# Attention inside a two-layer expert kernel: five TensorE visits a step in place of eight, and the outer product by head

## The reference

```python
for t in range(S):                                   # B, H, S, D = 4, 8, 768, 48
    cur = einsum('bhd,bhe->bhde', u * k[t], v[t])
    y[t] = einsum('bhd,bhde->bhe', r[t], state + cur)
    state = w[t][..., None] * state + einsum('bhd,bhe->bhde', k[t], v[t])
x = y.transpose(0, 2, 1, 3).reshape(B * S, H * D)    # 3072 x 384
h = x @ w_in;  x = (h * clip(h + 3, 0, 6) / 6) @ w_out     # d_ff = 2048
h = x @ w_in2; x = (h / (1 + exp(-h))) @ w_out2
```

## Time and profile before

| | |
|---|---|
| median of the runs | 945.53 us |
| the profiled execution | 945.16 us, its span 943.4 us |
| PE busy | 916.1 us (97%) |
| PEld, DVE, ACT, POOL busy | 84%, 49%, 33%, 16% |
| mean granted clock of TensorE | 0.978 |
| of the chain that ended last | PE 93%, DVE 2% |

### The profile page before, as it was taken

The page is one execution under the profiler, slowest core; times in us unless marked ns, Lnnn a source line. Parts: engine busy times, 40 slices in busy tenths (PEclk is TensorE's granted clock), DMA queues, the critical chain, the costliest instruction groups (busy, mean ns, idle before and its releaser), DMA issues.

```text
span 943.4 us, 14944 instructions
## 1 busy us (share of the span) xinstructions
PE 916.1 (97%) x5684; PEld 788.7 (84%) x5684; DVE 457.7 (49%) x692; ACT 313.9 (33%) x517; POOL 148.8 (16%) x134
## 2 busy tenths in 40 slices
PE   5679999999999999999999999999999999999998
PEld 4568888888888888888888789999999999999997
DVE  6866646564664656466445643333333333343332
ACT  2343223233223323332244542333332332332332
POOL 6454213321421332142000000000000000000000
PEclk7679999999999999999999999999999999999999
DMA  7561130304113030311203100000000000000000
GB/s 239 189 175 56 56 98 12 109 0 109 54 54 88 20 109 0 109 54 54 100 1 101 67 1 0 15 19 0 33 0 0 33 0 0 33 0 0 34 1 34
DMA packets 13367, 48.54 MB, mean 51 GB/s; under 512 B 1568, under 2 KB 2208, under 8 KB 13344
## 3 DMA queue, kind: packets, MB, share of 16 engines
q1 hardware_dynamic: 13344, 48.23, 16.3%
HBM read 43.50 MB, written 4.72 MB: 51 GB/s over the span
## 4 chain that ended last, share of the span: by engine, by line
PE 93%; DVE 2%; DMA 1%; POOL 1%; issue 1%; ACT 0%; SPq 0%; POOLq 0%; ACTq 0%
PE bank L652 15%; PE bank L653 14%; PE bank L654 14%; PE bank L676 7%; PE bank L678 7%; PE bank L677 7%; PE bank L664 7%; PE bank L666 7%; PE bank L665 7%; PE bank L706 2%; PE bank L732 2%; PE bank L716 2%; PE bank L736 1%; DMA x<-u_row 1%; PE bank L698 1%
## 5 line engine op out<-in xcount | busy, mean ns | idle before, releaser
L652 PE MATMUL bank<-x_hi,w_hi 128*128 (+1 forms) x576 | 230.0, 399 | 1.4 <-DVE x_lo L563 1.4
L654 PE MATMUL bank<-x_hi,w_lo 128*128 (+1 forms) x576 | 227.1, 394 | 0.0
L653 PE MATMUL bank<-x_lo,w_hi 128*128 (+1 forms) x576 | 227.0, 394 | 0.0
L375 ACT CAST g_hi<-g 128x512 fp32r<-128x512 f32 x192 | 119.1, 620 | 286.3 <-PE bank L678 144.3
L491 DVE TENSOR_TENSOR g<-g,bank 128x512 f32<-128x512 f32 x96 | 66.0, 687 | 244.4 <-ACT g L369 244.4
L498 DVE TENSOR_TENSOR g_lo<-g,g_hi 128x512 fp32r<-128x512 f32 x192 | 138.3, 720 | 0.9 <-ACT g_hi L375 0.9
L493 DVE SCALAR_TENSOR_TENSOR g<-g,bank 128x512 f32<-128x512 f32 x96 | 66.0, 688 | 141.3 <-ACT g L367 141.3
L652 PEld LDWEIGHTS bank<-x_hi,w_hi 128*128 128x128 f32 x576 | 108.8, 189 | 27.2 <-issue 4.0
L678 PE MATMUL bank<-w_hi,g_lo 128*128 128x384 f32 x384 | 129.5, 337 | 0.0
L676 PE MATMUL bank<-w_hi,g_hi 128*128 128x384 f32 x384 | 129.5, 337 | 0.0
L677 PE MATMUL bank<-w_lo,g_hi 128*128 128x384 f32 x384 | 128.9, 336 | 0.0
(11 more groups left out here) (89 smaller groups left out, 817.6 us busy)
## 6 DMA issues: line engine op xcount, KB each, us to landing
unit_in<-rkv_tm SPq DMA_DIRECT2D x23, 576.0 KB, 6.5
unit_in<-rk_fm SPq DMA_DIRECT2D x23, 448.0 KB, 4.1
x<-w SPq DMA_DIRECT2D x8, 768.0 KB, 4.9
unit_in<-w SPq DMA_DIRECT2D x8, 768.0 KB, 4.4
unit_in<-w_fm SPq DMA_DIRECT2D x23, 226.2 KB, 2.9
out<-tmp SPq DMA_DIRECT2D x5, 768.0 KB, 3.3
out<-tmp SPq DMA_DIRECT2D x4, 192.0 KB, 2.0
x<-rkv_tm SPq DMA_DIRECT2D x1, 576.0 KB, 12.7
```

The lines of the kernel that those rows point to most:

```text
L375: nc.scalar.copy(g_hi[:, p, :], g[:, p, :]).then_inc(ghi_done, 1)
L652: nc.tensor.matmul(h_ps[j % 2][:, :], wh, xh, start=k == 0, stop=False)
L653: nc.tensor.matmul(h_ps[j % 2][:, :], wh, xl, start=False, stop=False)
L654: last = nc.tensor.matmul(h_ps[j % 2][:, :], wl, xh, start=False, stop=k == KT - 1)
```

## The change

The pieces get names, and two that held two things are parted: transposes (TURN) and scores (SCORES), outer product (OUTER) and values (VALUES). `RUN_SLOTS` gives way to `VISITS = [3, 6, 9, 12, 14]`. Visit 0 does transposes and scores of unit 0. Visits 1 to 3 (the middle visits) do the transposes of unit b, outer product and values of unit b-1, and then the scores of unit b. Visit 4 does outer product and values of unit 3. The two scans of a unit stand in the slot ahead of its visit, its row sums in the visit. The transposes share `att[1]` with scores, the outer product shares `att[0]` with scores, the output has `att[2]`. Scores therefore wait for the copied keys (`kt_kept`) and for the addition of unit b-1's outer product to its state (`added`), and that addition now waits for the state's last read (`state_read`). On GpSimd the two products come behind decayed keys and queries; a one-column multiplication (`spin`) takes the waits ahead of the diagonal. The outer product is 8 matmuls of 48 columns, even heads at partitions 0 to 47 and odd heads at 64 to 111, in place of 4 of 96 over 112 rows, half of whose results were not used. The prologue keeps its order, apart from the outer product's form.

```diff
@@ -121,7 +122,7 @@
...
-        run_banks = [[att[0], att[1], att[2], att[2], att[0]]]
+        run_banks = [[att[0], att[1], att[0], att[1], att[2]]]
         pro_banks = [att + bank[3:5], bank[0:3] + bank[3:5]]
...
@@ -204,9 +207,13 @@
...
+        SCAN, FORWARD, OWN, TURN, SCORES, MASK, OUTER, VALUES, STATE, XHI, XLO = range(11)
+
         def pro_pieces(slot):
-            order = ([(0, 0), (0, 5), (1, 0), (1, 5)] if slot == 0 else
-                     [(slot - 1, 4), (slot - 1, 1), (slot - 2, 2), (slot - 2, 3), (slot + 1, 0), (slot + 1, 5)])
+            order = ([(0, SCAN), (0, FORWARD), (1, SCAN), (1, FORWARD)] if slot == 0 else
+                     [(slot - 1, OWN), (slot - 1, TURN), (slot - 1, SCORES), (slot - 1, MASK),
+                      (slot - 2, OUTER), (slot - 2, VALUES), (slot - 2, STATE), (slot - 2, XHI), (slot - 2, XLO),
+                      (slot + 1, SCAN), (slot + 1, FORWARD)])
             return [(b, k) for b, k in order if 0 <= b < B]
...
@@ -216,10 +223,17 @@
...
-        RUN_SLOTS = {0: 2, 4: 2, 5: 3, 1: 4, 2: 5, 3: 5}
+        VISITS = [3, 6, 9, 12, 14]
         def run_pieces(slot):
-            return [(b, k) for k, first in RUN_SLOTS.items() for b in range(B) if slot == 3 * b + first]
+            pieces = []
+            if slot in VISITS:
+                b = VISITS.index(slot)
+                pieces = [(b, OWN), (b, TURN), (b - 1, OUTER), (b - 1, VALUES), (b - 1, STATE), (b, SCORES), (b - 1, XHI), (b - 1, XLO), (b, MASK)]
+            elif slot + 1 in VISITS:
+                b = VISITS.index(slot + 1)
+                pieces = [(b, SCAN), (b, FORWARD)]
+            return [(b, k) for b, k in pieces if 0 <= b < B]
...
@@ -327,11 +341,10 @@
...
-            def queries_and_diagonal(b, a, c):
+            def old_diagonal_read(b, a, c):
                 pool.wait_ge(own_done, a + 1)
                 pool.wait_ge(y_full, a)
-                decayed_queries(b, a, c)
-                own_diagonal(b, a, c)
+                nc.gpsimd.tensor_tensor(spin[:, :], half[:, :], half[:, :], ALU.mult).then_inc(spun, 1)
...
@@ -352,9 +365,11 @@
...
                 for b in range(B):
+                    decayed_keys(b, B * (c + 1) + b, c)
+                    decayed_queries(b, B * (c + 1) + b, c)
                     own_products(b, B * (c + 1) + b, c)
-                    decayed_keys(b, B * (c + 1) + b, c)
-                    queries_and_diagonal(b, B * (c + 1) + b, c)
+                    old_diagonal_read(b, B * (c + 1) + b, c)
+                    own_diagonal(b, B * (c + 1) + b, c)
...
@@ -512,22 +527,22 @@
...
                     p_last = segs(back)[:, :, 0:1]
-                    if k == 0:
+                    if k == SCAN:
                         dve.wait_ge(w_loaded[m], 16 * taken(b, c))
...
                         if c is not None:
-                            dve.wait_ge(scaled, 2 * (a - B))
+                            dve.wait_ge(masked, 2 * a)
                         nc.vector.tensor_tensor_scan(back[:, ::-1], w[:, 1:WSEG][:, ::-1], back_add[:, ::-1], 0.0,
...
                         nc.vector.reciprocal(segs(fwd_add[:, :])[:, :, 0:1], p_last).then_inc(start_done, 1)
-                    if k == 5:
+                    if k == FORWARD:
                         dve.wait_ge(start_done, a + 1)
                         nc.vector.tensor_tensor_scan(fwd[:, :], w[:, 0:PAIRS * SEG], fwd_add[:, :], 0.0, ALU.mult, ALU.add).then_inc(fwd_done, 1)
-                    if k == 1:
+                    if k == MASK:
                         dve.wait_ge(diag_done, a + 1)
...
@@ -538,27 +553,27 @@
...
                                                       banks[q][:, :].rearrange("p (h t) -> p h t", h=4)).then_inc(masked, 1)
-                    if k == 4:
+                    if k == OWN:
                         dve.wait_ge(rku_done, a + 1)
...
                                              tm[:, 0, :].rearrange("p (i q d) -> p i q d", i=PAIRS, q=2), AX.X).then_inc(own_done, 1)
-                    if k == 2:
+                    if k == STATE:
                         if c is None:
...
                         else:
-                            dve.wait_ge(y_full, a + 1)
+                            dve.wait_ge(state_read, a - B + 1)
                             dve.wait_ge(scaled, 2 * (a - B) + 2)
-                        outer = banks[2][:, 0:PAIRS * 2 * D].rearrange("p (i e) -> p i e", i=PAIRS)
+                        outer = banks[2][:, 0:PAIRS * D].rearrange("p (i e) -> p i e", i=PAIRS)
                         for odd in range(2):
...
                             if c is None:
-                                nc.vector.tensor_copy(st, outer[rows, :, cols]).then_inc(added, 1)
+                                nc.vector.tensor_copy(st, outer[rows, :, :]).then_inc(added, 1)
                             else:
-                                nc.vector.tensor_tensor(st, st, outer[rows, :, cols], ALU.add).then_inc(added, 1)
-                    if k == 3:
+                                nc.vector.tensor_tensor(st, st, outer[rows, :, :], ALU.add).then_inc(added, 1)
+                    if k == XLO:
                         dve.wait_ge(xhi_done, a + 1)
...
@@ -688,18 +703,20 @@
...
                     rk, w, tm = units[m]
-                    if k == 1:
+                    if k == TURN:
                         pe.wait_ge(kt_done, a + 1)
                         if sets == 1:
-                            pe.wait_ge(added, 2 * a)
+                            pe.wait_ge(masked, 2 * a)
                         elif a > 0:
...
                         last.then_inc(kt_turned, 1)
+                    if k == SCORES:
                         pe.wait_ge(rt_done, a + 1)
                         if sets == 1:
-                            pe.wait_ge(xlo_done, a)
+                            pe.wait_ge(kt_kept, a + 1)
+                            pe.wait_ge(added, 2 * a)
                         for h in range(H):
...
@@ -707,15 +724,20 @@
...
                                 last.then_inc(scores_full, 1)
-                    if k == 2:
+                    if k == OUTER:
                         pe.wait_ge(kt_kept, a + 1)
-                        if some(2 * (a + 1 - sets)):
+                        if sets == 1:
+                            pe.wait_ge(masked, 2 * a + 2)
+                        elif a + 1 > sets:
                             pe.wait_ge(added, 2 * (a + 1 - sets))
                         pe.wait_ge(tm_loaded[m], 16 * taken(b, c))
-                        for i in range(PAIRS):
-                            last = nc.tensor.matmul(banks[2][0:KROWS, i * 2 * D:(i + 1) * 2 * D], kt_tok[:, i * KROWS:(i + 1) * KROWS],
-                                                    tm[:, 2, i * 2 * D:(i + 1) * 2 * D], start=True, stop=True)
+                        for h in range(H):
+                            q, i = h % 2, h // 2
+                            last = nc.tensor.matmul(banks[2][ODD * q:ODD * q + D, i * D:(i + 1) * D],
+                                                    kt_tok[:, i * KROWS + ODD * q:i * KROWS + ODD * q + D],
+                                                    tm[:, 2, h * D:(h + 1) * D], start=True, stop=True)
                         last.then_inc(outer_full, 1)
+                    if k == VALUES:
                         x_bank = banks[4]
...
@@ -729,7 +751,8 @@
...
                                 i, e = n // 3, n % 3 * Q
-                                nc.tensor.matmul(region(n), state[b][0:KROWS, i, e:e + Q], rk[:, 0, i, :], start=n < 4, stop=False)
+                                last = nc.tensor.matmul(region(n), state[b][0:KROWS, i, e:e + Q], rk[:, 0, i, :], start=n < 4, stop=False)
+                            last.then_inc(state_read, 1)
                         for n in range(REGIONS):
...
```

More of the change, by code:

```diff
@@ L74, in build @@
         half = sb("half", [P, 1])
+        spin = sb("spin", [P, 1])
         def x2_step(c, k):
@@ L150, in build @@
         scaled = sem("scaled")
+        state_read = sem("state_read")
         added = sem("added")
@@ L164, in build @@
         diag_done = sem("diag_done")
+        spun = sem("spun")
         v_mid_done = sem("v_mid_done")
@@ L406, in attention @@
                         nc.scalar.copy(v_mid_put[b % 2], middle.rearrange("p i (q e) -> p i q e", q=2)).then_inc(v_mid_done, 1)
-                    if k == 3:
+                    if k == XHI:
                         act.wait_ge(y_full, a + 1)
```

## The result

The changed kernel takes 983.15 us (median of 4 runs, 981.89 to 985.09) against 946.18 us: a ratio of 1.0394, 95% interval 1.0365 to 1.0423, slower. The forecast was 985 in a range of 955 to 1000. The profiled execution has a span of 980.3 us, and of the chain that ended last TensorE now holds 78% where it held 93%.

The account below looks back on a forecast made before the run. TensorE bounds the kernel, so attention costs the time TensorE spends on it. A step adds 3 x 1.58 + 1.09 - 0.22 = 5.61 us, five 28.0, on 945.16 gives 973.2; 12 for the clock gives 985, range 955 to 1000.

Parts of the forecast that it names:

- Three exits a step: Delays of the dense matmuls behind an attention visit on TensorE, taken at 0.16 us each; joining visits removes three a step.
- The term of 0.028 a record: Outer product: 0.028 us per narrow record, from the values' rows, so 16 take 0.45; a gain beyond 0.45 was excluded.
- T: Zero point of the forecast's times: the end of `sums1` in the visit's slot.
- 4.42: TensorE's cost in us of one attention unit in the kernel before: 1.57 + 2.53 + 0.32.
- Each station: Chain before middle-visit scores: backward scan, keys, forward scan, queries, `g_lo`, two products, row sums, additions; scores at T + 4.75.
- the scan's meeting with the keys: VectorE's forward scan, held up by GpSimd's decayed keys on the shared port pair, ends 1.09 us behind them.
- The meetings of `g_lo` with queries and product: `g_lo` on VectorE ends 0.54 us after GpSimd's queries; the first product takes 1.43 and ends 0.86 after `g_lo`.
- two rows: Clock evidence: 2.8 us of standing before 45.40 brought clock 0.50; a 0.7 us pause at 539 left it 1.00.
- The clock kept at 973: Rival 1: the same waits with TensorE's clock kept, 973 us (968 to 978); chance 0.26.
- harmless meetings at 953: Rival 2: the two port-pair meetings don't lengthen the chain, 1.5 us a step, 953 (949 to 960); chance 0.13.
- the clock lost nearly everywhere: Rival 4: clock lost in nearly every visit or slow to return, 24 to 33 us over 973, 997 to 1006; chance 0.09.
- The faster side: Rival 3: additions come in time for scores, 937 us, or 941 with visit 0's copy waited for; chance 0.07.

Follow-up runs that it names:

- the outer product alone: The kernel before with only the outer product's new form, 8 matmuls of 48 columns in two column halves: 940.26 us, 0.9937.
- two experiments from different sides: Changed kernel with products ahead of keys and queries again: 944.45 us; changed kernel with backward scans of units 1 to 3 a slot earlier: 944.03 us.
- a third: Changed kernel with GpSimd's decayed keys in the loop cut to one column per pair: 958.23 us, 1.0122.
- The filled pause: Changed kernel with seven more matmuls of 512 columns in each middle visit, ahead of the wait for the addition: 970.21 us, 1.0252.
- unit 0's own bank alone: Changed kernel with only the transposes of unit 0 moved to `att[2]`, so its scores skip the wait for the keys' copy: 982.05 us, 1.0377.
- joined, no pause: Changed kernel with visits in slots 4, 7, 10, 13, 14, backward scans two slots ahead, forward scans one, unit 0's transposes in `att[2]`: 938.66 us, 0.9923.

## Why the prediction was right

**What it saves.** Three exits a step and the outer product. The last visit saved 0.29 and not 0.22 (the same 0.29 a unit as with the outer product alone): L736 to L754 is 0.49 with the change of tiles, where I had 0.55, and the 0.09 for the entry came as forecast. The term of 0.028 a record was taken from 128-column streams; with 48 columns it is about (0.49 - 0.10) / 16 = 0.024. By that the bound I had excluded (faster than 0.028) was crossed.

**The middle visits.** Forecast 1.58 us more for each, without the clock: scores at T + 4.75. Measured: the visits end 5.69 after T on average with 0.14 to 0.15 behind, 5.84 in all, 1.42 more than 4.42. Each station was in its place. The additions ended at T + 4.45 in the visit shown, 0.25 ahead of the forecast: 0.13 by the second product (0.87 for 1.00) and 0.12 along the way to it. (The forecast's own terms add up to T + 4.75 for their end, not 4.70; row sums and additions overlap by about as much in the trace.) Of this, 0.10 is given back because scores start 0.15 behind the additions and not 0.05. That the products' place decides is shown by two experiments from different sides, that the scan's meeting with the keys lengthens the chain, by a third: without it the scores came 0.82 us earlier on average. The meetings of `g_lo` with queries and product were only read from the trace, where their ends fit to 0.02 us.

**Visit 0.** Forecast 1.09, measured 2.49 + 0.17 + 0.15 (a late `g_lo` two slots on, in four of the five turns) against 1.73: 1.08. For the masks it took 2.3 us, where its rows give 2.2 and the trace has 2.15.

**The clock.** Forecast: half of the 15 visits at 1.6 us. Measured: 8, at 5.8 - 4.2 = 1.6. The filled pause gives the same 12.9 us by itself. This was the term with the widest bounds (0 to 33), and that it fell in the middle was a guess between two rows; the loss doesn't go by the pause's length (a visit with scores at T + 4.40 lost the clock, one with T + 4.72 kept it). The count is the profiled run's. The mean granted clock of the four runs is 0.964 to 0.969 and lowest in the two slowest, so it was probably not 8 in each; with unit 0's own bank alone it was 7 of 15. The size was a choice too: the clock was at 0.50 in both rows from 45.40 to 51.80, and the forecast priced one of them; behind the middle visit shown it was at 0.50 for one such stretch, 88.40 to 91.60.

**The sum.** 15 x 1.42 + 5 x 1.08 - 5 x 0.29 + 8 x 1.6 = 38.1 us, and the five turns of the loop show just 38.1. The start of the loop was 1.1 us earlier than in the trace of before, which makes 980.4 for a span of 980.3. Forecast were 28.0 + 12 = 40.

**Joined visits.** The prediction gave the three exits 0.48 us a step; the expectations of later runs held that the change of tile shapes takes this back. By the steps 81.91 (separate, outer product by head) and 81.64 (joined, no pause) joining is worth 0.26 us a step, 1.3 us in 938. What takes the rest back is not the tiles: a middle visit takes 3.88 us where the two separate ones take 1.57 + 2.17 = 3.74, and this 0.14 lies between values and scores (1.82 for 1.67), where the scores stand behind the additions. So a joined visit spares an exit (0.14) and a late entry (0.09) and gives 0.14 back: 3 x 0.09 = 0.27 a step. That the wait for the additions is the cause of the 0.14 is read from the traces; no experiment took it away. At best the outer product's form is 5.7 us of the gain and the whole idea 7.0 (five steps each).

**The rivals.** The clock kept at 973, harmless meetings at 953, and the clock lost nearly everywhere are out by the runs above. The faster side was not to be had with scans and products placed as they were. A chain started a slot earlier took the pauses of the middle visits away (944.0), and 938.7 needed unit 0's own bank and evenly spaced visits as well.

## What to carry to other kernels

A change that joins work on the busiest engine also joins its inputs' deadlines: write down, for each thing that the joined visit waits for, when its whole chain can start and what stands ahead of it in each queue. Here one line of order in a queue that is busy 16% of the time cost 38.7 us, because TensorE waited for VectorE, VectorE for GpSimd's products, and these stood behind instructions that waited for VectorE, and because a pause of under 2 us was paid a second time through the clock. Price parts of a change apart: one of them, alone in the old kernel, was worth 6 us.

## What the runs showed of the hardware

TensorE lost half its clock behind 8 of 15 pauses of 1.7 to 2.0 us, behind none of 15 of about 1.05 us, and behind none when the same time was filled with matmuls.

VectorE's instructions with two SBUF inputs end a fixed time behind the GpSimd instruction that they meet: 1.08 to 1.09 us for the forward scan, whether it starts 0.1 or 1.4 us behind it, and 0.54 to 0.56 us for `g_lo`. When `g_lo` and GpSimd's next instruction both waited, `g_lo` ended first in each of the 20 visits of the changed kernel where they met, by 0.86 to 0.87 us. It is no rule: in the kernel before, GpSimd went first twice, where `g_lo` came only 0.14 us ahead of the end of the running instruction (L320, until 89.26):

```profile
89.22 1.01 POOL L314 TENSOR_TENSOR unit_in<-unit_in 128x384 f32<-128x384 f32 x1
```

```profile
89.12 1.67 DVE L498 TENSOR_TENSOR g_lo<-g,g_hi 128x512 fp32r<-128x512 f32 x1
```

A 48-column matmul record in column halves costs 0.024 us on average. At a change of tile shape the next matmul starts about 0.10 us later than within a stream (0.191 between the last record of L716 and the first of L732, where L716's own stand 0.098 apart). Scores started 0.15 us behind the end of the additions in every middle visit of every kernel here but that with the filled pause.
